# Last two attention levels in smaller places taken by ScalarE, and level halves paired in one half slot

## The chip, the cores and the metric

The kernel runs on one core of one Trainium2 chip. The metric is the device time in microseconds (us) of one execution, the median of several runs. TensorE (PE) multiplies matrices, VectorE (DVE), ScalarE (ACT) and GpSimd (POOL) work elementwise, SyncE (SP) issues the transfers. Each engine takes its instructions in the order in which they are written and waits for semaphores that the other engines raise.

## The reference, cut to what matters

```python
# attention: batch 4, heads 8, seq 768, head_dim 48
f = 1.0 / (1.0 + np.exp(-f_logit))
for t in range(S):
    state = f[:, :, t, :, None] * state + np.einsum('bhd,bhe->bhde', k[:, :, t], v[:, :, t])
    y[:, :, t] = np.einsum('bhd,bhde->bhe', q[:, :, t], state)
# x = y as 3072 tokens x 384; first network, d_ff 2048
h = x @ w_in
g = np.where(h >= 1, h, np.where(h <= -1, 0.0, (h + 1) ** 2 / 4))
x = g @ w_out
# second network, d_ff 1536
g = x @ w_gate
out = (g * sigmoid(g) * (x @ w_val)) @ w2_out
```

All tensors are fp32. The two networks are done with three fp32r products for each fp32 product (hi times hi, hi times lo, lo times hi).

## The kernel before, in words

**Attention.** The sequence is cut into 6 units of 128 steps. The gated recurrence inside a unit is unrolled into a 128x128 matrix of scores for each head, filled in seven levels (`LEVELS`, m = 1, 2, 4 to 64). At level m the queries in the right half of every block of 2m steps meet the keys in its left half. Then the queries of the right half are multiplied by the running gate product (`scale_q`, L731, VectorE), the keys of the left half likewise (`scale_k`, L892, GpSimd), and the gate products of the two halves are merged (`merge`, L900, GpSimd). The 16 pairs of heads go in two groups of 8, so a level has two steps and a unit has 14 (`STEPS`), numbered 0 to 13.

**One step, before.** ScalarE copies the queries of the right halves into `right_q`, one copy for each head of a pair, with zeros between (`copy_right`, L546, two copies of 64x512). TensorE multiplies them with the keys into one PSUM bank of three (`level`, L344, for level 64 L348). VectorE moves the bank into `scores` (`take_level`): for levels 1 to 32 by two masked copies (COPY_PREDICATED, L748), for level 64 by eight small copies (L755). After the levels come four outputs (`outputs`, L370 to L381), and for all units but the last the transposed keys (`turn_keys`, L389), the new state (`key_values`, L400). TensorE may refill a bank when the engine that takes it has done so (`free`).

**The networks.** Unit m of the first network has 16 chunks. A chunk is `hidden` (9 matmuls of 128x512, L431 to L433) and, two chunks later (`LAG`), `project1` (9 matmuls, L445 to L447). Between them VectorE clamps (`clamp`, L818), ScalarE squares (L604), VectorE takes the maximum (`activate`, L825), ScalarE rounds the result to fp32r (`split_g1`, g_hi, L611), and GpSimd subtracts that from it (g_lo, L932). `project1` waits for g_hi and g_lo of its chunk; `hidden(c)` waits until `activate(c-2)` is done.

**The order.** It is written by hand. A chunk c has two half slots: h = 2c lies between `hidden(c)` and the `project1` beside it, h = 2c + 1 behind it. A `Plan` gives the half slots in which each piece of a unit's attention is issued. Unit 0 (`FIRST`) runs alone ahead of the networks, unit 1 (`SECOND`) in unit 0 of the first network, units 2 to 5 (`USUAL`) in its units 1 to 4. Preparations (`own`, `diag`, `place`, `sigmoid`, `gated`) stand in negative half slots, inside the unit before. On VectorE a chunk is: attention of h = 2c, `activate(c-1)`, `clamp(c)`, attention of 2c + 1. On GpSimd: attention of 2c, `split_g1(c-1)`, attention of 2c + 1. The unit of the second network that follows has no attention.

Of the kernel before, what the change touches and what calls it, by code (L numbers as in the profile page):

```python
# [27 lines left out]
STEPS = 2 * NL  # L28
# [9 lines left out]
Y0 = STEPS  # L38
# [12 lines left out]
Plan = namedtuple("Plan", "own diag place sigmoid gated step last_merge y y_out tk tk_out kv state state_place")  # L51
USUAL = Plan(own=(-9, -8), diag=(-8, -7), place=(-6, -5, -4, -3), sigmoid=(-2, -1), gated=(-1, 0),
             step=(1, 3, 5, 7, 8, 9, 10, 12, 13, 14, 15, 17, 18, 19), last_merge=21,
             y=(21, 21, 22, 22), y_out=(21, 22, 22, 23), tk=(23, 23, 24, 24), tk_out=(24, 24, 25, 25),
             kv=25, state=26, state_place=27)
SECOND = Plan(own=(-9, -8), diag=(-8, -7), place=(0, 2, 3, 4), sigmoid=(3, 4), gated=(4, 5),
              step=(6, 8, 9, 10, 11, 12, 13, 14, 16, 17, 18, 19, 20, 21), last_merge=22,
              y=(23, 23, 24, 24), y_out=(23, 24, 24, 25), tk=(25, 25, 26, 26), tk_out=(26, 26, 27, 27),
              kv=27, state=28, state_place=29)
FIRST = USUAL._replace(diag=(-3, -2), sigmoid=(-3, -2), gated=(-3, -2))  # L60
# [7 lines left out]
def steps_at(a, h):  # L68
    return [s for s in range(STEPS) if PLANS[a].step[s] == h]
# [19 lines left out]
def merges(a, s):  # L89

    return sum(STEPS if 0 < b < UNITS - 1 else STEPS - 2 for b in range(a)) + s


def build(nc, f, q, k, qt, kt, v, w_in, w_out, w_gate, w_val, w2_out, masks, ident, x1, out):
# [51 lines left out]
    mask = att("mask", [P, (NL - 1) * HALF // 2], I32)  # L146
# [72 lines left out]
    def _(sp):  # L219
# [71 lines left out]
        sp.wait_ge(dve_took, (UNITS - 1) * DVE_A_UNIT + STEPS)  # L291
# [20 lines left out]
    def _(pe):  # L312
        def free(a, i):

            j = i - 3
            if j < 0:
                a, j = a - 1, FILLS + j
            if a < 0:
                return
            if j < STEPS:  # L320
                pe.wait_ge(dve_took, a * DVE_A_UNIT + j + 1)
            elif j < TK0:
                pe.wait_ge(x_lo_done, a * B + j - Y0 + 1)
# [8 lines left out]
        def level(a, s):  # L332
            li, g = s // 2, s % 2
            free(a, s)
            pe.wait_ge(q_copied, a * STEPS + s + 1)
            if li:
                pe.wait_ge(k_scaled, a * STEPS + s - 1)
            else:
                pe.wait_ge(k_in[g], 16 * (a + 1))
            for x in range(BP // 2):  # L340
                bp = g * BP // 2 + x
                if li < NL - 1:
                    for half in range(2):
                        last = pe.matmul(of(a, s)[rows(half), x * R:(x + 1) * R],  # L344
                                         keys[:, bp, half * HALF:(half + 1) * HALF],
                                         right_q[:, bp, half].rearrange("p e t -> p (e t)"), start=True, stop=True)
                else:
                    last = pe.matmul(of(a, s)[rows(x % 2), x // 2 * P:(x // 2 + 1) * P], keys[:, bp, 0:HALF],  # L348
                                     right_q[:, bp].rearrange("p s e t -> p (s e t)"), start=True, stop=True)
            last.then_inc(filled, 1)  # L350

        def outputs(a, b):
            i = Y0 + b
            free(a, i)
            pe.wait_ge(dve_took, a * DVE_A_UNIT + STEPS - 1 + b // 2)
            if b == 0:
                pe.wait_ge(v_in, 16 * (a + 1))
# [24 lines left out]
            last.then_inc(filled, 1)  # L382

        def turn_keys(a, b):
            i = TK0 + b
            free(a, i)
            pe.wait_ge(k_scaled, a * STEPS + STEPS - 1 + b // 2)
# [16 lines left out]
        def attention(a, h):  # L404
            for s in steps_at(a, h):
                level(a, s)
            for b in range(B):
                if PLANS[a].y[b] == h:
                    outputs(a, b)
# [101 lines left out]
    def _(act):  # L511
# [16 lines left out]
        def copy_right(a, s):  # L528
            li, g = s // 2, s % 2
            act.wait_ge(q_scaled, a * SCALED_A_UNIT + s + 1)  # L530
            if li:
                act.wait_ge(filled, fill(a, s - 1))
            elif a > 0:
                act.wait_ge(filled, fill(a - 1, STEPS))
            for e in range(2):
                o = group(right_q, g)[rows(e), :, :, e, :]
                i = group(queries, g)[rows(e)]
                if li < NL - 1:
                    m = LEVELS[li]
                    i = i.rearrange("p x (h b s r) -> p (x h) b s r", h=2, s=2, r=m)[:, :, :, 1, :]  # L540
                    o = o.rearrange("p x h (b r) -> p (x h) b r", r=m)
                    if m == 1:
                        i, o = i[:, :, :, 0], o[:, :, :, 0]
                else:
                    i = i[:, :, HALF:P].rearrange("p x (s t) -> p x s t", s=2)
# [23 lines left out]
        def attention(a, h):  # L569
# [6 lines left out]
            for s in steps_at(a, h + 1):  # L576
                copy_right(a, s)
            for b in range(B):
                if PLANS[a].y_out[b] == h:
                    split_y(a, b)  # L580
            if a < UNITS - 1:
                for b in range(B):
                    if PLANS[a].tk_out[b] == h:
                        take_keys(a, b)
# [114 lines left out]
    def _(dve):  # L699
# [33 lines left out]
        def take_level(a, s):  # L733
# [9 lines left out]
            if li < NL - 1:  # L743
                m = LEVELS[li]
                for half in range(2):
                    o = group(scores, g)[rows(half), :, :, half * HALF:(half + 1) * HALF]
                    o = o.rearrange("p x e (b s r) -> p (x e) b s r", s=2, r=m)[:, :, :, 1, :]
                    last = dve.copy_predicated(o, level_mask(li, half),  # L748
                                               t[rows(half), :].rearrange("p (x b r) -> p x b r", x=BP, r=m))
            else:  # L750
                for e in range(2):
                    o = group(scores, g)[rows(0), e::2, :, HALF:P].rearrange("p x e (s t) -> p x s e t", s=2)
                    i = t[rows(e), :].rearrange("p (x s e t) -> p x s e t", s=2, e=2, t=HALF // 2)
                    for x in range(BP // 4):
                        last = dve.tensor_copy(o[:, x], i[:, x])  # L755
            last.then_inc(dve_took, 1)

        def decay_state(a):
            dve.wait_ge(g_merged, merges(a, STEPS))
# [22 lines left out]
        def attention(a, h):  # L782
# [7 lines left out]
            for s in steps_at(a, h - 1):  # L790
                take_level(a, s)
            for s in steps_at(a, h):
                scale_q(a, s)
            if h == PLANS[a].last_merge and 0 < a < UNITS - 1:
# [4 lines left out]
            for b in range(B):  # L799
                if PLANS[a].y_out[b] == h:  # L800
                    split_y(a, b)
# [72 lines left out]
    def _(pool):  # L874
# [6 lines left out]
        def scale_k(a, s):  # L881
            li, g = s // 2, s % 2
            m = LEVELS[li]
            pool.wait_ge(filled, fill(a, s + 1))
            if li:
                pool.wait_ge(g_merged, merges(a, s - 1))
                pool.wait_ge(k_scaled, a * STEPS + s - 1)
# [14 lines left out]
        def attention(a, h):  # L902
# [64 lines left out]
def _constants():  # L967
# [4 lines left out]
    for m in LEVELS[:-1]:  # L972
# [62 lines left out]
```

## Time and profile before

| | |
|---|---|
| median of 3 runs | 1078.5 us (1078.38 to 1078.94) |
| the profiled execution's own time | 1078.47 us |
| its span | 1076.7 us |
| PE, share of the span | 94% |
| DVE, ACT, POOL | 51%, 41%, 42% |
| TensorE clock granted, mean | 0.979 |

The span is from the first to the last recorded instruction. Unit 0 of attention lies at about 16 to 78 us. The units 1 to 5 lie beside the first network until about 558 us, then the first network's last unit and the second network follow without attention. A matmul in fp32 is recorded as two passes, so one level step of 16 matmuls shows as x32. A matmul's recorded length includes a tail in which the next one already runs, so what a matmul costs is read from the distance between starts.

### The profile page before, as it was taken

Reading aid. Unit: us, or ns where it says so; the run is one execution under the profiler, and the core shown is the slowest. Engines: PE = TensorE matmul, PEld = TensorE weight load, DVE = VectorE, ACT = ScalarE, POOL = GpSimd, SP = SyncE. Lnnn points to the kernel's source line nnn. Section 1 sums busy time; section 2 is a strip of 40 time slices with the busy share of each in tenths; the row PEclk is TensorE's granted clock in tenths of the full one; section 3 lists DMA queues with packets and bytes.
Section 4 is the critical chain, followed back from the end, with each engine's and each line's share of the span. In section 5 each row is a group of like instructions: output and inputs, shape, how many; then the busy total and the mean of one; then the engine's idle time right before and its main releaser. Section 6 shows DMA issues by size and latency. Waiting matters only on the chain.

```text
span 1076.7 us, 19206 instructions
## 1 busy us (share of the span) xinstructions
PE 1015.5 (94%) x7816; PEld 828.8 (77%) x7816; DVE 547.0 (51%) x745; ACT 445.2 (41%) x808; POOL 450.8 (42%) x368
## 2 busy tenths in 40 slices
PE   2477899999999999999999999999999999999997
PEld 2465677778778777877788888888888888888886
DVE  7965965884686488568736532223222222222221
ACT  3439538544753855375336532122222222222221
POOL 3956962763564476447327422121221212212121
PEclk9569999999999999999999999999999999999999
DMA  9423005003300600220043110010010010000000
GB/s 357 158 72 145 1 2 216 31 2 124 122 1 2 216 30 2 82 107 2 2 177 131 45 39 22 1 59 1 1 59 1 1 59 1 30 1 1 30 1 29
DMA packets 17367, 63.52 MB, mean 59 GB/s; under 512 B 1920, under 2 KB 2176, under 8 KB 16512
## 3 DMA queue, kind: packets, MB, share of 16 engines
q1 hardware_dynamic: 17280, 62.30, 15.8%
q8 instruction: 62, 1.02, 0.4%
q14 instruction: 25, 0.20, 0.1%
HBM read 52.85 MB, written 9.44 MB: 58 GB/s over the span
## 4 chain that ended last, share of the span: by engine, by line
PE 83%; issue 5%; DVE 5%; ACT 3%; POOL 3%; DMA 1%; SPq 0%; POOLq 0%; ACTq 0%; DVEq 0%
PE acc L445 10%; PE acc L447 10%; PE acc L446 10%; PE bank L473 7%; PE bank L471 7%; PE bank L472 7%; PE hid L431 6%; PE bank L344 5%; PE hid L432 5%; PE hid L433 5%; DVE scores L748 3%; PE hid L473 2%; PE hid L472 2%; PE hid L471 2%; PE bank L376 2%
## 5 line engine op out<-in xcount | busy, mean ns | idle before, releaser
L939 POOL TENSOR_TENSOR g_lo<-prod,g_hi 128x512 fp32r<-128x512 f32 x72 | 93.1, 1293 | 347.4 <-ACT g_hi L650 347.4
L932 POOL TENSOR_TENSOR g_lo<-act_tmp,g_hi 128x512 fp32r<-128x512 f32 x96 | 140.5, 1463 | 188.8 <-ACT g_hi L611 188.8
L837 DVE TENSOR_TENSOR sig<-sig,bank 128x512 f32<-128x512 f32 x72 | 49.6, 688 | 275.9 <-ACT sig L644 275.9
L748 DVE COPY_PREDICATED scores<-mask,bank 64x512 f32<-64x512 int32 x144 | 134.2, 932 | 28.4 <-PE bank L344 26.6
L650 ACT CAST g_hi<-prod 128x512 fp32r<-128x512 f32 x72 | 44.9, 624 | 247.6 <-PE acc L447 247.6
L892 POOL TENSOR_TENSOR keys<-keys,gates 128x512 f32<-128x512 f32 x82 | 110.2, 1343 | 44.1 <-PE bank L344 32.7
L611 ACT CAST g_hi<-act_tmp 128x512 fp32r<-128x512 f32 x96 | 59.6, 621 | 164.1 <-DVE act_tmp L825 164.1
L344 PEld LDWEIGHTS bank<-right_q,keys 128*64 128x64 f32 x2304 | 81.0, 150 | 58.8 <-issue 54.6
L344 PE MATMUL bank<-right_q,keys 128*64 128x64 f32 x2304 | 91.0, 238 | 36.0 <-ACT right_q L546 28.1
L445 PE MATMUL acc<-g_hi,wout_hi 128*128 128x512 f32 x288 | 117.0, 406 | 8.0 <-POOL g_lo L932 8.0
L431 PE MATMUL hid<-x_hi,win_hi 128*128 128x512 f32 x288 | 119.0, 413 | 4.0 <-DVE act_tmp L825 4.0
L546 ACT COPY right_q<-queries 64x512 f32<-64x512 f32 x168 | 105.8, 630 | 40.7 <-DVE queries L731 22.5
L433 PE MATMUL hid<-x_hi,win_lo 128*128 128x512 f32 x288 | 113.1, 393 | 0.0
L432 PE MATMUL hid<-x_lo,win_hi 128*128 128x512 f32 x288 | 113.0, 393 | 0.0
L446 PE MATMUL acc<-g_lo,wout_hi 128*128 128x512 f32 x288 | 112.7, 391 | 0.0
L447 PE MATMUL acc<-g_hi,wout_lo 128*128 128x512 f32 x288 | 112.5, 391 | 0.0
L731 DVE TENSOR_TENSOR queries<-queries,gates 128x512 f32<-128x512 f32 x84 | 88.3, 1051 | 2.2 <-ACT right_q L546 0.5
L825 DVE TENSOR_TENSOR act_tmp<-hid,act_tmp 128x512 f32<-128x512 f32 x96 | 66.1, 689 | 41.3 <-ACT act_tmp L604 39.8
L445 PE MATMUL acc<-g_hi,wo_hi 128*128 128x512 f32 x216 | 84.1, 389 | 0.2 <-POOL g_lo L939 0.2
L446 PE MATMUL acc<-g_lo,wo_hi 128*128 128x512 f32 x216 | 84.0, 389 | 0.0
L471 PE MATMUL bank<-x_hi,wg_hi 128*128 128x512 f32 x216 | 84.0, 389 | 0.0
L472 PE MATMUL bank<-x_lo,wg_hi 128*128 128x512 f32 x216 | 84.0, 389 | 0.0
(80 smaller groups left out, 1851.6 us busy)
## 6 DMA issues: line engine op xcount, KB each, us to landing
gates<-in_f_dram SPq DMA_DIRECT2D x12, 512.0 KB, 5.3
queries<-in_q_dram SPq DMA_DIRECT2D x12, 512.0 KB, 5.4
keys<-in_k_dram SPq DMA_DIRECT2D x12, 512.0 KB, 4.7
values<-in_v_tok_dram SPq DMA_DIRECT2D x6, 1024.0 KB, 8.8
q_tok<-in_q_tok_dram SPq DMA_DIRECT2D x12, 384.0 KB, 8.6
k_tok<-in_k_tok_dram SPq DMA_DIRECT2D x12, 384.0 KB, 9.0
x_dram<-x_out SPq DMA_DIRECT2D x6, 768.0 KB, 3.9
x_raw<-x_dram SPq DMA_DIRECT2D x6, 768.0 KB, 5.5
```

The lines of the kernel that those rows point to most:

```text
L344: last = pe.matmul(of(a, s)[rows(half), x * R:(x + 1) * R], keys[:, bp, half * HALF:(half + 1) * HALF], right_q[:, bp, half].rearrange("p ...
L431: pe.matmul(o, hi, x_hi[m % 2][:, kc], start=(kc == 0), stop=False)
L432: pe.matmul(o, hi, x_lo[m % 2][:, kc], start=False, stop=False)
L433: last = pe.matmul(o, lo, x_hi[m % 2][:, kc], start=False, stop=(kc == KC - 1))
L445: pe.matmul(o, hi, g_hi[:, c % RING], start=first, stop=False)
L446: pe.matmul(o, hi, g_lo[:, c % RING], start=False, stop=False)
L447: last = pe.matmul(o, lo, g_hi[:, c % RING], start=False, stop=last_chunk)
L471: pe.matmul(o[c % 2][:, :], hi, x_hi[u % 2][:, kc], start=(kc == 0), stop=False)
L472: pe.matmul(o[c % 2][:, :], hi, x_lo[u % 2][:, kc], start=False, stop=False)
L748: last = dve.copy_predicated(o, level_mask(li, half), t[rows(half), :].rearrange("p (x b r) -> p x b r", x=BP, r=m))
L892: pool.tensor_tensor(kl, kl, right.broadcast_to([P, BP // 2 * P // (2 * m), m]), ALU.mult).then_inc(k_scaled, 1)
L932: pool.tensor_tensor(g_lo[:, c % RING, :], act_tmp[:, 2 + c % 2, :], g_hi[:, c % RING, :].bitcast(F32), ALU.subtract).then_inc(g_lo_done, 1)
```

## The change

Three things change together.

1. **Level 32 in one place** (`whole`). Both groups of heads go into one bank, with only the 32 left keys of each half as weights (32 columns), four column quarters side by side. No mask is needed, and ScalarE takes the bank by four copies of 32 rows (`take_whole`).
2. **Level 64 without `right_q`** (`last_level`). Each head is its own matmul with 64 rows of keys and the queries read directly, into two banks. ScalarE takes them by two copies each (`take_last`). The two copies of the queries for each step are gone, and `scale_q` and `scale_k` of these two steps wait for the matmuls.
3. **The order.** A plan names copies, takes, scalings and GpSimd work apart. For units 2 to 5 steps 0 and 1 stand in one half slot (2), 2 and 3 in 5, 4 and 5 in 8, 6 and 7 in 11, 8 and 9 in 13; level 32 is in 16 and level 64 in 18. The outputs begin at 21 as before. `merge` no longer waits for `scale_q`.

TensorE's 14 blocks of levels for a unit from the third on become 7, unit 1's become 12, with the networks' matmuls between.

```diff
-USUAL = Plan(own=(-9, -8), diag=(-8, -7), place=(-6, -5, -4, -3), sigmoid=(-2, -1), gated=(-1, 0),
-             step=(1, 3, 5, 7, 8, 9, 10, 12, 13, 14, 15, 17, 18, 19), last_merge=21,
+ALONE = usual((1, 3, 5, 7, 8, 9, 10, 12, 13, 14), 16, 18, 21)
+USUAL = usual((2, 2, 5, 5, 8, 8, 11, 11, 13, 13), 16, 18, 21,
+              copy=(0, 1, 3, 4, 6, 7, 9, 10, 12, 12, 15, 15), take=(3, 4, 6, 7, 9, 10, 12, 13, 14, 15))
+SECOND = usual((6, 8, 9, 10, 11, 12, 13, 14, 16, 17), 19, 21, 23, place=(0, 2, 3, 4), sigmoid=(3, 4), gated=(4, 5))
...
+        def whole(a):
+
+            free(a, WHOLE0)
+            pe.wait_ge(q_copied, (a + 1) * COPIES)
+            pe.wait_ge(k_scaled, a * SCALES + STEPS)
+            for x in range(BP):
+                for half in range(2):
+                    q = 2 * half + x % 2
+                    last = pe.matmul(of(a, WHOLE0)[Q * q:Q * (q + 1), x // 2 * R:(x // 2 + 1) * R],
+                                     keys[:, x, half * HALF:half * HALF + Q],
+                                     right_q[:, x, half].rearrange("p e t -> p (e t)"), start=True, stop=True)
+            last.then_inc(filled, 1)
+
+        def last_level(a):
+
+            for e in range(2):
+                free(a, LAST0 + e)
+            pe.wait_ge(q_scaled, a * SCALED_A_UNIT + SCALES)
+            pe.wait_ge(k_scaled, a * SCALES + SCALES - 2)
+            for x in range(BP):
+                for e in range(2):
+                    last = pe.matmul(of(a, LAST0 + e)[rows(x % 2), x // 2 * HALF:(x // 2 + 1) * HALF],
+                                     keys[rows(e), x, 0:HALF], queries[rows(e), x, HALF:P], start=True, stop=True)
+            last.then_inc(filled, 2)
...
+        def take_whole(a):
+            act.wait_ge(filled, fill(a, LAST0))
+            act.wait_ge(dve_took, a * DVE_A_UNIT + STEPS)
...
+                    last = act.copy(o, i)
+            last.then_inc(act_took, 1)
+
+        def take_last(a, e):
+            act.wait_ge(filled, fill(a, Y0))
+            act.wait_ge(dve_took, a * DVE_A_UNIT + STEPS)
...
         def scale_q(a, s):
...
-            dve.wait_ge(q_copied, a * STEPS + s + 1)
+            if s < COPIES:
+                dve.wait_ge(q_copied, a * COPIES + s + 1)
+            else:
+                dve.wait_ge(filled, fill(a, Y0))
...
         def scale_k(a, s):
...
-            pool.wait_ge(filled, fill(a, s + 1))
+            if s < STEPS:
+                pool.wait_ge(filled, fill(a, s + 1))
+            else:
+                pool.wait_ge(filled, fill(a, LAST0 if s < COPIES else Y0))
...
         def merge(a, s):
...
-            pool.wait_ge(k_scaled, a * STEPS + s + 1)
-            pool.wait_ge(q_scaled, a * SCALED_A_UNIT + 2 + s + 1)
+            pool.wait_ge(k_scaled, a * SCALES + s + 1)
```

On GpSimd, at the first level of unit 2 (L892 and L954 are `scale_k`, L900 and L961 `merge`, L932 and L993 the g_lo of a chunk). Before:

```order
L892 TENSOR_TENSOR keys<-keys,gates 128x512
L900 TENSOR_TENSOR gates<-gates 128x512
L932 TENSOR_TENSOR g_lo<-act_tmp,g_hi 128x512
L892 TENSOR_TENSOR keys<-keys,gates 128x512
L900 TENSOR_TENSOR gates<-gates 128x512
L932 TENSOR_TENSOR g_lo<-act_tmp,g_hi 128x512
```

And now:

```order
L954 TENSOR_TENSOR keys<-keys,gates 128x512
L961 TENSOR_TENSOR gates<-gates 128x512
L954 TENSOR_TENSOR keys<-keys,gates 128x512
L961 TENSOR_TENSOR gates<-gates 128x512
L993 TENSOR_TENSOR g_lo<-act_tmp,g_hi 128x512 x2
```

Both scalings and both merges stand ahead of the g_lo of the chunk.

On VectorE, at the last levels of unit 2 (L731 and L798 are `scale_q`, L748 the masked and L755 the plain take, L825 and L884 `activate`, L818 and L877 `clamp`). Before:

```order
L825 TENSOR_TENSOR act_tmp<-hid,act_tmp 128x512
L818 TENSOR_SCALAR act_tmp<-hid 128x512
L731 TENSOR_TENSOR queries<-queries,gates 128x16x32
L748 COPY_PREDICATED scores<-mask,bank 64x16x32 x2
L731 TENSOR_TENSOR queries<-queries,gates 128x8x64
L825 TENSOR_TENSOR act_tmp<-hid,act_tmp 128x512
L818 TENSOR_SCALAR act_tmp<-hid 128x512
L755 COPY scores<-bank 64x2x2x32 x8
L731 TENSOR_TENSOR queries<-queries,gates 128x8x64
L755 COPY scores<-bank 64x2x2x32 x8
L825 TENSOR_TENSOR act_tmp<-hid,act_tmp 128x512
```

And now:

```order
L798 TENSOR_TENSOR queries<-queries,gates 128x16x32 x2
L884 TENSOR_TENSOR act_tmp<-hid,act_tmp 128x512
L877 TENSOR_SCALAR act_tmp<-hid 128x512
L798 TENSOR_TENSOR queries<-queries,gates 128x8x64 x2
L884 TENSOR_TENSOR act_tmp<-hid,act_tmp 128x512
L877 TENSOR_SCALAR act_tmp<-hid 128x512
```

The takes are gone from here, and both scalings of level 64, which now wait for its matmuls, stand ahead of an `activate`.

## Rows read from the trace of the kernel before

**Rows 1.** Busy time of stretches; columns: stretch, length, busy us by engine.

```profile
17.00:76.00 59.00, 33.63 (x568) 30.52 (x564) 51.82 (x62) 26.75 (x42) 45.93 (x36) 0.65 0.38 147
278.60:374.60 96.00, 95.01 (x1009) 75.93 (x1008) 67.93 (x98) 53.94 (x108) 52.91 (x47) 1.00 0.20 70
648.00:1076.00 428.00, 423.19 (x1866) 349.77 (x1864) 102.60 (x142) 99.10 (x160) 89.22 (x69) 1.00 0.05 17
```

**Rows 2.** What PE waited for in 182.5 to 278.6 us: total, times, longest.

```profile
PE acc L445 <- POOL g_lo L932: 1.0, 2, 0.6
```

**Rows 3.** PE in order of time, levels of unit 3: start, us, line, tile.

```profile
301.93 1.15 PE L344 MATMUL bank<-right_q,keys 128*64 128x64 f32 x32
303.01 0.50 PE L445 MATMUL acc<-g_hi,wout_hi 128*128 128x512 f32 x1
...
305.28 1.15 PE L344 MATMUL bank<-right_q,keys 128*64 128x64 f32 x32
...
308.62 1.15 PE L344 MATMUL bank<-right_q,keys 128*64 128x64 f32 x32
...
314.01 1.15 PE L344 MATMUL bank<-right_q,keys 128*64 128x64 f32 x32
```

**Rows 4.** PE in order of time, level 64, outputs, state of unit 3.

```profile
336.07 1.09 PE L348 MATMUL bank<-right_q,keys 128*64 128x128 f32 x16
...
342.95 0.84 PE L370 MATMUL bank<-queries,state_apart 128*32 128x128 f32 x24
343.61 0.84 PE L376 MATMUL bank<-scores,values 128*32 128x128 f32 x24
...
358.23 2.07 PE L400 MATMUL bank<-values,keys_tok 128*64 128x48 f32 x64
```

**Rows 5.** Chain of waits, 350 to 360 us: start, us on the chain.

```profile
352.42 0.87 PE bank L389 x8
```

**Rows 6.** POOL in order of time, unit 3.

```profile
284.04 1.53 POOL L892 TENSOR_TENSOR keys<-keys,gates 128x512 f32<-128x512 f32 x1
285.65 1.04 POOL L900 TENSOR_TENSOR gates<-gates 128x512 f32<-128x512 f32 x1
...
303.18 1.28 POOL L892 TENSOR_TENSOR keys<-keys,gates 128x512 f32<-128x512 f32 x1 [0.77 <-PE bank L344]
304.54 0.66 POOL L900 TENSOR_TENSOR gates<-gates 128x128 f32<-128x128 f32 x1
305.15 1.28 POOL L932 TENSOR_TENSOR g_lo<-act_tmp,g_hi 128x512 fp32r<-128x512 f32 x1
...
333.97 1.06 POOL L892 TENSOR_TENSOR keys<-keys,gates 128x512 f32<-128x512 f32 x1 [1.88 <-PE bank L348]
335.11 0.22 POOL L900 TENSOR_TENSOR gates<-gates 128x8 f32<-128x8 f32 x1
335.29 1.75 POOL L932 TENSOR_TENSOR g_lo<-act_tmp,g_hi 128x512 fp32r<-128x512 f32 x1
```

**Rows 7.** DVE in order of time, unit 3.

```profile
283.62 2.68 DVE L748 COPY_PREDICATED scores<-mask,bank 64x512 f32<-64x512 int32 x2 [0.70 <-PE bank L344]
...
332.18 0.69 DVE L731 TENSOR_TENSOR queries<-queries,gates 128x512 f32<-128x512 f32 x1
332.90 0.69 DVE L825 TENSOR_TENSOR act_tmp<-hid,act_tmp 128x512 f32<-128x512 f32 x1
...
335.81 1.77 DVE L731 TENSOR_TENSOR queries<-queries,gates 128x512 f32<-128x512 f32 x1
```

**Rows 8.** ACT groups by line: count, busy, mean ns.

```profile
L611 ACT CAST g_hi<-act_tmp 128x512 fp32r<-128x512 f32 x96 | 59.6, 621 | 164.1 <-DVE act_tmp L825 164.1
...
L556 ACT COPY keys_tok<-bank 128x512 f32<-128x512 f32 x20 | 10.7, 588 | 3.2 <-PE bank L389 3.1
```

**Rows 9.** PE in order of time, end of unit 0.

```profile
53.85 1.97 PE L344 MATMUL bank<-right_q,keys 128*64 128x64 f32 x32 [0.98 <-issue]
56.61 1.97 PE L348 MATMUL bank<-right_q,keys 128*64 128x128 f32 x16 [0.79 <-ACT right_q L546]
63.40 1.98 PE L348 MATMUL bank<-right_q,keys 128*64 128x128 f32 x16 [4.82 <-POOL keys L892]
67.37 1.51 PE L376 MATMUL bank<-scores,values 128*32 128x128 f32 x24 [2.00 <-DVE queries L731]
```

**Rows 10.** DVE, ACT and POOL in order of time, end of unit 0.

```profile
55.26 1.48 DVE L748 COPY_PREDICATED scores<-mask,bank 64x512 f32<-64x512 int32 x2
...
63.84 1.81 DVE L755 COPY scores<-bank 64x128 f32<-64x128 f32 x8
...
52.50 1.25 ACT L546 COPY right_q<-queries 64x512 f32<-64x512 f32 x2 [0.84 <-DVE queries L731]
...
56.44 3.57 POOL L879 TENSOR_TENSOR q_tok<-q_tok,k_tok 128x768 f32<-128x768 f32 x2
```

More of the change, by code:

```diff
@@ L33 @@
 PIECE = 2 * DM
-Y0 = STEPS
+WHOLE0 = STEPS
+LAST0 = WHOLE0 + 1
+Y0 = LAST0 + 2
 TK0 = Y0 + B
@@ L65, with placed @@
 Q = P // 4
-def steps_at(a, h):
-    return [s for s in range(STEPS) if PLANS[a].step[s] == h]
+def placed(places, h):
+    return [i for i, p in enumerate(places) if p == h]
 def turns(m, h):
@@ L89, in merges @@
 def merges(a, s):
-    return sum(STEPS if 0 < b < UNITS - 1 else STEPS - 2 for b in range(a)) + s
+    return sum(SCALES if 0 < b < UNITS - 1 else SCALES - 2 for b in range(a)) + s
 def build(nc, f, q, k, qt, kt, v, w_in, w_out, w_gate, w_val, w2_out, masks, ident, x1, out):
@@ L341, in level @@
                 bp = g * BP // 2 + x
[L342 to L349, printed above, removed]
-            last.then_inc(filled, 1)
+                for half in range(2):
+                    last = pe.matmul(of(a, s)[rows(half), x * R:(x + 1) * R],
+                                     keys[:, bp, half * HALF:(half + 1) * HALF],
+                                     right_q[:, bp, half].rearrange("p e t -> p (e t)"), start=True, stop=True)
+            last.then_inc(filled, 1)
+        def whole(a):
[3 more added lines that the diff above has]
+            for x in range(BP):
+                for half in range(2):
+                    q = 2 * half + x % 2
[13 more added lines that the diff above has]
+            last.then_inc(filled, 2)
         def outputs(a, b):
@@ L404, in attention @@
         def attention(a, h):
-            for s in steps_at(a, h):
+            for s in placed(PLANS[a].step, h):
                 level(a, s)
-            for b in range(B):
-                if PLANS[a].y[b] == h:
-                    outputs(a, b)
+            if h == PLANS[a].whole:
+                whole(a)
+            if h == PLANS[a].last:
+                last_level(a)
+            for b in placed(PLANS[a].y, h):
+                outputs(a, b)
             if a < UNITS - 1:
@@ L533, in copy_right @@
             elif a > 0:
-                act.wait_ge(filled, fill(a - 1, STEPS))
+                act.wait_ge(filled, fill(a - 1, LAST0))
             for e in range(2):
[L536 to L545, printed above, removed]
+                o = group(right_q, g)[rows(e), :, :, e, :].rearrange("p x h (b r) -> p (x h) b r", r=m)
+                i = group(queries, g)[rows(e)].rearrange("p x (h b s r) -> p (x h) b s r", h=2, s=2, r=m)[:, :, :, 1, :]
+                if m == 1:
+                    i, o = i[:, :, :, 0], o[:, :, :, 0]
                 last = act.copy(o, i)
             last.then_inc(q_copied, 1)
+        def take_whole(a):
+            act.wait_ge(filled, fill(a, LAST0))
+            act.wait_ge(dve_took, a * DVE_A_UNIT + STEPS)
+            t = bank[fill(a, WHOLE0) % 3]
+            for half in range(2):
+                for par in range(2):
+                    q = 2 * half + par
+                    o = scores[half * HALF:half * HALF + Q, par::2, :, half * HALF + Q:(half + 1) * HALF]
+                    i = t[Q * q:Q * (q + 1), :].rearrange("p (x e t) -> p x e t", e=2, t=Q)
+                    last = act.copy(o, i)
[3 more added lines that the diff above has]
+            act.wait_ge(dve_took, a * DVE_A_UNIT + STEPS)
+            t = bank[fill(a, LAST0 + e) % 3]
+            for par in range(2):
+                last = act.copy(scores[rows(0), par::2, e, HALF:P], t[rows(par), :].rearrange("p (x t) -> p x t", t=HALF))
+            last.then_inc(act_took, 1)
         def take_keys(a, b):
@@ L575, in attention @@
                     sigmoid(a, g)
-            for s in steps_at(a, h + 1):
+            if h == PLANS[a].whole_take:
+                take_whole(a)
+            if h == PLANS[a].last_take:
+                for e in range(2):
+                    take_last(a, e)
+            for s in placed(PLANS[a].copy, h):
                 copy_right(a, s)
-            for b in range(B):
-                if PLANS[a].y_out[b] == h:
-                    split_y(a, b)
+            for b in placed(PLANS[a].y_out, h):
+                split_y(a, b)
             if a < UNITS - 1:
-                for b in range(B):
-                    if PLANS[a].tk_out[b] == h:
-                        take_keys(a, b)
+                for b in placed(PLANS[a].tk_out, h):
+                    take_keys(a, b)
                 if h == PLANS[a].state_place:
@@ L742, in take_level @@
                 dve.wait_ge(mask_in, 16)
[L743 to L755, printed above, removed]
+            m = LEVELS[li]
+            for half in range(2):
+                o = group(scores, g)[rows(half), :, :, half * HALF:(half + 1) * HALF]
+                o = o.rearrange("p x e (b s r) -> p (x e) b s r", s=2, r=m)[:, :, :, 1, :]
+                last = dve.copy_predicated(o, level_mask(li, half),
+                                           t[rows(half), :].rearrange("p (x b r) -> p x b r", x=BP, r=m))
             last.then_inc(dve_took, 1)
         def decay_state(a):
-            dve.wait_ge(g_merged, merges(a, STEPS))
+            dve.wait_ge(g_merged, merges(a, SCALES))
             dve.wait_ge(state_placed, 2 * a)
@@ L789, in attention @@
                     gated(a, g)
-            for s in steps_at(a, h - 1):
+            for s in placed(PLANS[a].take, h):
                 take_level(a, s)
-            for s in steps_at(a, h):
+            for s in placed(PLANS[a].scale, h):
                 scale_q(a, s)
-            if h == PLANS[a].last_merge and 0 < a < UNITS - 1:
+            if h == PLANS[a].decay and 0 < a < UNITS - 1:
                 decay_state(a)
@@ L798, in attention @@
                     add_state(a, g)
-            for b in range(B):
-                if PLANS[a].y_out[b] == h:
-                    split_y(a, b)
+            for b in placed(PLANS[a].y_out, h):
+                split_y(a, b)
         def split_w2(i):
@@ L971, in _constants @@
     parts = []
-    for m in LEVELS[:-1]:
+    for m in LEVELS[:-2]:
         right = i[:, (i[0] // m) % 2 == 1]
```

56 lines of the change are left out of this document (32 added, 24 removed).

## The prediction, made before the result was known

> **What bounds the kernel now.** I read the busy time by stretches first. Where attention and the first network run together, TensorE is busy 95.01 of 96.00 us; in the second network 423.19 of 428.00; only unit 0 of attention, at 17 to 76 us, has it busy 33.63 of 59.00, at a granted clock of 0.65, with VectorE at 51.82 [rows 1]. So there are two kernels in one: a start bound by VectorE and the chain through it, and a long stretch in which every microsecond that TensorE's order needs is a microsecond of the end. Then I read what TensorE waits for in a usual unit: 1.0 us in two waits for g_lo of GpSimd [rows 2]. Engines other than TensorE cost there only if they make it wait, and each of them has room on average. TensorE's own sequence came next [rows 3 to 5], last the engines that release it [rows 6 to 8].
>
> **Switching blocks on TensorE.** Two levels with 9 large matmuls between start 305.28 - 301.93 = 3.35 us apart, with 18 between 314.01 - 308.62 = 5.39, so 9 large matmuls cost 2.04 and a level in its place 1.31. From its start to the next large matmul it is 303.01 - 301.93 = 1.08 [rows 3]. The other 0.23 us is paid for going from one kind of matmul to the other and back, once for a block. Two levels side by side should pay it once. That is this change's gain: 7 blocks fewer in each of units 2 to 5, 7 x 4 x 0.23 = 6.4 us, and 2 fewer in unit 1, 0.5 us. Together -6.9 us.
>
> The trace shows a price for the switch. The Trainium skill's page "TensorEngine Tiling (Array Packing)", Key Properties, says that a change of tiling mode drains the engine while another tile of the same mode does not; by that rule too the price goes with the block, and the trace agrees (0.23 us).
>
> **The matmuls themselves.** A level step is 32 passes in 1.08 us, 34 ns each [rows 3]. Level 32 was 2 x 1.08 = 2.16 us and is now 64 passes of 32 columns. The nearest rows with 32 columns are 24 passes in 343.61 - 342.95 = 0.66 us, 27 ns [rows 4], so 1.7 to 2.2 us; I take no change. Level 64 was 2 steps of x16; the row of one is 1.09 with its tail [rows 4], so about 2.1 us for both. It is now 64 passes of 64 rows by 64 columns. Narrow passes of x64 took 2.07 us [rows 4], 31 to 34 ns each whatever they hold, so 2.0 to 2.2: no change. What the trace doesn't show is whether two matmuls on different row halves and the same columns overlap. If not, each costs half of a full pass of 128 columns (0.87 / 8 = 109 ns [rows 5]), 54 ns, so 64 x 54 = 3.5 us, +1.4 a unit; that is the upper end. If four quarters ran wholly side by side, 64 x 13.6 = 0.9 us, -1.2 a unit, the lower end. I take the middle since that is where rows of narrow passes lie.
>
> **Unit 0, alone.** VectorE loses four takes, about 2 x 1.48 + 2 x 1.81 = 6.6 us [rows 10]. I don't count them as gain, for other things become late. `whole` needs the copies of steps 10 and 11; the second comes after `scale_q` of step 9, as in the row that ends at 52.50 + 1.25 = 53.75 [rows 10]. At that stretch's clock a pass costs 1.97 / 32 = 62 ns [rows 9], so 64 passes end at 53.75 + 3.9 = 57.7. Then GpSimd scales keys for both groups (2 x (1.06 + 0.22) = 2.6, to 60.3), for the last level waits for it [rows 6]; the level takes 3.9 (64.2), and ScalarE's four copies 4 x 0.59 = 2.4 [rows 8], so the outputs may start at 66.6, against 67.37 [rows 9]: -0.8 us. In the same place GpSimd's two products of 3.57 us for unit 1 [rows 10] are now split around step 10, and VectorE's sum of the second stands before `scale_q` of step 12; that ends by about 66.4 as well, so it's no later. Bounds: at full clock both blocks are 2.2 instead of 3.9 us, -4 us; if row halves don't overlap at this clock, +2.9 more.
>
> **What the change makes late in units 2 to 5.** Three places. I set each against the time at which TensorE would arrive.
>
> *Half slot 2.* GpSimd does `scale_k`, `merge`, `scale_k`, `merge` ahead of g_lo of chunk 0. From the end F of step 0: 2 x (1.53 + 1.04 + 0.08 between) = 5.3, then g_lo 1.28 [rows 6], with 0.1 for the handing over: F + 6.7. TensorE after F: step 1 and project with its switch 3.35 - 0.08, then `hidden(2)` 2.04: F + 5.3. It waits 1.4 us. Before, one `scale_k` and one `merge` stood there. The scalings took 1.53 beside masked copies (2.68 us [rows 7]) and 1.06 to 1.28 elsewhere [rows 6]; by 1.28 the wait is 0.9. Upper end 1.7, by a g_lo of 1.6. Queued behind the late project are the pair of slot 5 and the rest of TensorE, so it is paid in full.
>
> *Half slot 8.* The same with 1.28 and 0.66: 2 x (1.28 + 0.66 + 0.08) + 1.28 + 0.1 = 5.4, against 5.3. Some scalings are longer here, so I take 0.3; ends 0 and 0.8. Slots 5, 11 and 13 are odd, there g_lo of the chunk stands ahead of the pair, and slot 16 has the level of slot 18 behind it before its project: nothing.
>
> *Half slot 18.* `scale_q` of steps 12 and 13 used to wait for copies only. Now they wait for the end L of level 64, and `activate(8)` is behind them, for which `hidden(10)` waits. TensorE gets there at L + 2.2 (one project and its switch). VectorE: 0.69 + 0.69 + 0.69 = 2.1 if undisturbed [rows 7]. But GpSimd starts `scale_k` at the same L. The trace shows what that does: `scale_q` took 1.77 us beside a g_lo of 1.75, and 0.69 alone [rows 6, 7]. With one of GpSimd's 1.06 between the two, `activate` ends at L + 3.1, so `hidden(10)` waits 0.9. Then ScalarE's rounding 0.62 [rows 8] and g_lo 1.28 give L + 5.5 where project comes at L + 5.2: 0.3 more. Together 1.2, ends 0 and 1.7. In unit 5 GpSimd has nothing to do for the last level, so only some 0.15 is left.
>
> The Trainium skill's "GPSIMD Engine Reference", Specifications, says that GpSimd shares its SBUF interfaces with VectorE and contends with VectorE instructions that have two SBUF inputs; `scale_q` has two. The rows agree (1.77 against 0.69 us). Without such contention slot 18 would cost near nothing and the sum would be some 3 us lower, so this rule speaks against the change.
>
> Sum of waits: 3 x (1.4 + 0.3 + 1.2) + (1.4 + 0.3 + 0.15) = 10.5 us. Removed: on GpSimd the wait of `merge` for `scale_q`, at nothing, for both engines were held by the same contention there. ScalarE gets 8 copies for 4; it has 42 us of room in 96 [rows 1], and its takes end before slot 21. The transfer of the masks is shorter, hidden.
>
> **Sum.** -6.9 - 0.8 + 10.5 = +2.8. The profiled execution took 1078.47 us, 0.03 under the median, so 1081.3.
>
> **Rivals.**
> *B, faster.* GpSimd is quicker now that the masked copies lie in other half slots: 1.28 for scalings, slot 8 free, slot 18 at 0.3. Then waits are 4 x 0.9 + 3 x 0.3 = 4.5, and the sum is -6.9 - 0.8 + 4.5 = -3.2: 1075.3. For it: scalings of 1.06 occur [rows 6]. Against: at levels 1 and 2 the masked copies still follow at once. It decides when the pair with its g_lo takes under 6.2 us instead of 6.7.
> *C, a wash.* The wait behind slot 2 is half of what I give it, since the scaling of one group may run before the masked copy beside it starts: -4 x 0.7, so 1078.5.
> *D, slower still.* The row halves of level 64 don't overlap: 5 x 1.4 + 2.9 = +9.9 on the forecast, 1091. For it: same columns one behind the other. Against: nothing shown.
> *E, the last level at a quarter.* 5 x -1.2 - 2 = -8: 1073. Against it the 31 ns floor of narrow passes [rows 4]. The Trainium skill's tiling page, Theoretical Speedup, allows four times where both dimensions are at most 64; this would be its effect.
> *F, no saving.* The 0.23 belongs to each bank filled, not to the block: 1081.3 + 6.9 = 1088. Against: x64 in one block took 2.07 [rows 4], no more for each pass than x32.
>
> **Chances.** Forecast 0.40, B 0.24, C 0.20, D 0.07, E 0.04, F 0.05. The range runs from 1073 to 1087. The forecast's own is 1079.5 to 1084. About 2.2 us (0.2%) is what a measurement can tell; the cases give faster 0.29, same 0.24, slower 0.47.
>
> **What will show it.** Right: pairs of levels as x64 in about 2.2 us; TensorE waiting for g_lo 1 to 1.6 us behind slot 2 of units 2 to 5 and for act_tmp behind level 64; unit 0's outputs starting at 66 to 67 us; a usual unit of about 97.4 us for 96.0. Wrong: a usual unit under 96; level 64's block far from 2.1 us; unit 0 shorter by over 3 us.

## The result and the profile after

The changed kernel took 1069.07 us (median of 6 runs, 1068.19 to 1070.0), the kernel before in the same comparison 1078.44 us. The ratio is 0.9912 with a 95% interval of 0.9899 to 0.9925: 0.9% faster. The prediction was 1081.3 us, slower, with a range from 1073 to 1087. The time lies outside it, on the other side.

The profiled execution took 1068.27 us (span 1066.5). First the busy time of the two stretches that answer to [rows 1], one usual unit being 94.92 us long where it was 96.0:

```profile
17.00:76.00 59.00, 31.12 (x642) 28.60 (x639) 46.97 (x44) 29.18 (x46) 46.73 (x36) 0.83 0.42 158
283.99:378.91 94.92, 91.65 (x1041) 74.04 (x1040) 59.47 (x78) 56.42 (x112) 51.41 (x47) 1.00 0.20 71
```

TensorE's busy time in a unit fell from 95.01 to 91.65 us, by 3.4, while the unit became only 1.1 shorter. So TensorE has less to do and waits more. What it waited for in one unit, 278 to 373 us (who, for whom, total, times, longest), against 1.0 us in [rows 2]:

```profile
PE acc L491 <- POOL g_lo L993: 2.7, 4, 1.5
PE hid L477 <- DVE act_tmp L884: 0.6, 1, 0.6
```

TensorE in order of time in that unit, against [rows 3, 4]. L364 is a level of two halves, L377 level 32 (`whole`), L390 level 64 (`last_level`), L491 a project and L477 a hidden; in brackets the idle time before and who ended it:

```profile
278.46 2.08 PE L364 MATMUL bank<-right_q,keys 128*64 128x64 f32 x64
280.47 0.50 PE L491 MATMUL acc<-g_hi,wout_hi 128*128 128x512 f32 x1
...
286.33 0.47 PE L491 MATMUL acc<-g_hi,wout_hi 128*128 128x512 f32 x1 [1.48 <-POOL g_lo L993]
...
303.60 0.47 PE L491 MATMUL acc<-g_hi,wout_hi 128*128 128x512 f32 x1 [0.25 <-POOL g_lo L993]
...
320.52 1.10 PE L377 MATMUL bank<-right_q,keys 128*32 128x64 f32 x64
321.55 0.50 PE L491 MATMUL acc<-g_hi,wout_hi 128*128 128x512 f32 x1
...
325.85 1.16 PE L390 MATMUL bank<-queries,keys 64*64 64x64 f32 x64
326.94 0.50 PE L491 MATMUL acc<-g_hi,wout_hi 128*128 128x512 f32 x1
...
329.89 0.50 PE L477 MATMUL hid<-x_hi,win_hi 128*128 128x512 f32 x1 [0.61 <-DVE act_tmp L884]
```

The three waits that the prediction placed are there: 1.48, 0.25 and 0.61 us, where it gave 1.4, 0.3 and 0.9. What it did not have is in the starts: level 32 takes 321.55 - 320.52 = 1.03 us for 64 passes, level 64 takes 326.94 - 325.85 = 1.09. That is 16 and 17 ns a pass, where the prediction took 31 to 34.

The wait behind slot 2 on GpSimd, both scalings (L954) and merges (L961) ahead of g_lo (L993), as the order said:

```profile
279.70 1.53 POOL L954 TENSOR_TENSOR keys<-keys,gates 128x512 f32<-128x512 f32 x1 [1.62 <-PE bank L364]
281.31 1.04 POOL L961 TENSOR_TENSOR gates<-gates 128x512 f32<-128x512 f32 x1
282.31 1.53 POOL L954 TENSOR_TENSOR keys<-keys,gates 128x512 f32<-128x512 f32 x1
283.91 1.04 POOL L961 TENSOR_TENSOR gates<-gates 128x512 f32<-128x512 f32 x1
284.91 1.27 POOL L993 TENSOR_TENSOR g_lo<-act_tmp,g_hi 128x512 fp32r<-128x512 f32 x1
```

The end of unit 0 on TensorE, against [rows 9]. The outputs (L419) start 2.1 us earlier (65.23 for 67.37), and the two small levels take some 1.9 us each at this place, not 3.9. The granted clock of 50 to 63 us is 0.50 (1.2 GHz) in both profiles:

```profile
53.62 1.94 PE L377 MATMUL bank<-right_q,keys 128*32 128x64 f32 x64 [5.60 <-ACT right_q L587]
59.36 1.99 PE L390 MATMUL bank<-queries,keys 64*64 64x64 f32 x64 [3.80 <-POOL keys L954]
65.23 1.51 PE L419 MATMUL bank<-scores,values 128*32 128x128 f32 x24 [3.89 <-DVE queries L798]
```

Not all of the 2.1 us is the change. The first block of levels, TensorE's first matmuls, starts at 16.36 us in the kernel before and at 15.81 in the changed one:

```profile
16.36 1.97 PE L344 MATMUL bank<-right_q,keys 128*64 128x64 f32 x32 [16.36 <-ACT right_q L546]
15.81 1.97 PE L364 MATMUL bank<-right_q,keys 128*64 128x64 f32 x32 [15.81 <-ACT right_q L587]
```

In the experiments below whose unit 0 is the changed kernel's (4 to 8) this start lies between 16.18 and 16.44 us. From it to the outputs it is 51.01 us before, 49.42 in the changed kernel and 49.40 to 49.47 in those five, so 1.6 us is what the change gives there, and 0.55 us is an earlier start that it doesn't explain.

By the starts of each unit's state (L400, L443), the 10.2 us between the two profiled executions are: unit 0 2.1 (75.60 to 73.51), unit 1 2.7 (94.87 to 92.19 us long), units 2 to 4 1.2 each, and what is left, 1.9, in unit 5 and behind it.

### The profile page after: what moved, and what is told of

Same layout as the page of the kernel before. It is cut to its first block, busy times and chain, and to the rows that moved or that the text cites. A ratio compares the mean times of both kernels' runs of the same rounds, so it can differ in the third digit from the quotient of the medians.

```text
span 1066.5 us, 19376 instructions
## 1 busy us (share of the span) xinstructions
PE 994.6 (93%) x8008; PEld 816.0 (77%) x8008; DVE 502.3 (47%) x625; ACT 458.4 (43%) x832; POOL 446.1 (42%) x368
## 4 chain that ended last, share of the span: by engine, by line
PE 78%; POOL 10%; issue 6%; ACT 3%; DVE 2%; DMA 1%; SPq 0%; POOLq 0%; ACTq 0%; DVEq 0%
PE acc L491 10%; PE acc L493 9%; PE acc L492 9%; PE bank L517 7%; PE bank L518 7%; PE bank L519 7%; PE hid L477 5%; PE hid L479 4%; PE hid L478 4%; POOL keys L954 4%; PE bank L364 4%; POOL g_lo L993 3%; PE hid L517 2%; PE hid L519 2%; PE hid L518 2%
## 5 line engine op out<-in xcount | busy, mean ns | idle before, releaser
L993 POOL TENSOR_TENSOR g_lo<-act_tmp,g_hi 128x512 fp32r<-128x512 f32 x96 | 134.0, 1397 | 166.8 <-ACT g_hi L675 166.8
L954 POOL TENSOR_TENSOR keys<-keys,gates 128x512 f32<-128x512 f32 x82 | 109.5, 1336 | 65.2 <-PE bank L364 43.8
L491 PE MATMUL acc<-g_hi,wout_hi 128*128 128x512 f32 x288 | 117.2, 407 | 14.8 <-POOL g_lo L993 14.8
L814 DVE COPY_PREDICATED scores<-mask,bank 64x512 f32<-64x512 int32 x120 | 116.1, 967 | 15.9 <-PE bank L364 14.4
L477 PE MATMUL hid<-x_hi,win_hi 128*128 128x512 f32 x288 | 116.9, 406 | 5.7 <-DVE act_tmp L884 5.7
L587 ACT COPY right_q<-queries 64x512 f32<-64x512 f32 x144 | 90.8, 631 | 43.9 <-PE bank L364 21.8
L364 PE MATMUL bank<-right_q,keys 128*64 128x64 f32 x1920 | 71.0, 236 | 32.2 <-ACT right_q L587 26.0
L364 PEld LDWEIGHTS bank<-right_q,keys 128*64 128x64 f32 x1920 | 65.5, 149 | 44.2 <-issue 41.4
L798 DVE TENSOR_TENSOR queries<-queries,gates 128x512 f32<-128x512 f32 x84 | 81.3, 995 | 29.9 <-PE bank L390 25.5
L884 DVE TENSOR_TENSOR act_tmp<-hid,act_tmp 128x512 f32<-128x512 f32 x96 | 65.9, 687 | 52.7 <-ACT act_tmp L668 51.6
L877 DVE TENSOR_SCALAR act_tmp<-hid 128x512 f32<-128x512 f32 x96 | 65.7, 685 | 47.0 <-PE hid L479 47.0
L491 PE MATMUL acc<-g_hi,wo_hi 128*128 128x512 f32 x216 | 84.1, 389 | 0.2 <-POOL g_lo L1000 0.2
L493 PE MATMUL acc<-g_hi,wo_lo 128*128 128x512 f32 x216 | 84.0, 389 | 0.0
```

What stands on the lines that cost most here:

```text
L364: last = pe.matmul(of(a, s)[rows(half), x * R:(x + 1) * R], keys[:, bp, half * HALF:(half + 1) * HALF], right_q[:, bp, half].rearrange("p ...
L477: pe.matmul(o, hi, x_hi[m % 2][:, kc], start=(kc == 0), stop=False)
L491: pe.matmul(o, hi, g_hi[:, c % RING], start=first, stop=False)
L493: last = pe.matmul(o, lo, g_hi[:, c % RING], start=False, stop=last_chunk)
L814: last = dve.copy_predicated(o, level_mask(li, half), t[rows(half), :].rearrange("p (x b r) -> p x b r", x=BP, r=m))
L954: pool.tensor_tensor(kl, kl, right.broadcast_to([P, BP // 2 * P // (2 * m), m]), ALU.mult).then_inc(k_scaled, 1)
```

## The experiments

Each kernel is the changed one with the edit shown. Its time stands beside the changed kernel's 1069.07; ratios are to the kernel before in the same comparison.

**1. Level 32 on one quarter after the other.**

```diff
-            for x in range(BP):
-                for half in range(2):
+            for half in range(2):
+                for x in (*range(0, BP, 2), *range(1, BP, 2)):
```

> Level 32 in all six units with its 32 matmuls in another order: eight in a row on the same quarter of the columns. Same instructions, same sizes. Theory A (a pass holds its quarter for about 64 ns, and the block takes 16 ns a pass only because four quarters run side by side): the block takes about 64 x 64 ns = 4.1 us for 1.03, +3.1 in five units and more in unit 0: about 1085. Theory B (a pass with 32 columns of weights is cheap in itself, by its short weight load): no change, 1069.

Measured 1080.72 us, ratio 1.002 (1.001 to 1.003): the whole gain is gone. The block on TensorE:

```profile
327.14 3.18 PE L377 MATMUL bank<-right_q,keys 128*32 128x64 f32 x64
330.25 0.50 PE L491 MATMUL acc<-g_hi,wout_hi 128*128 128x512 f32 x1
```

It takes 3.11 us, 49 ns a pass, for the same instructions in another order. A unit is 96.9 us for 94.9. Theory B falls. Theory A stands, with a pass of 49 ns instead of my 64, so four quarters side by side gave three times, not four.

**2. Level 64 on one half of the rows after the other.**

```diff
-            for x in range(BP):
-                for e in range(2):
+            for e in range(2):
+                for x in range(BP):
                     last = pe.matmul(of(a, LAST0 + e)[rows(x % 2), x // 2 * HALF:(x // 2 + 1) * HALF],
```

> Level 64 in all units with its 32 matmuls in another order: first all on rows 0 to 63, then all on rows 64 to 127, so that only two of the four quarters of the array follow each other. Theory A (side by side is what makes it cheap): the block costs 32 ns a pass as the levels of two halves do, 2.0 us for 1.09, +0.9 in five units and up to 1.8 in unit 0, of which units 2 to 4 hide nothing: about 1074. Theory B (64 rows of weights instead of 128 are cheap in themselves): no change, 1069.

Measured 1073.03 us (0.9955, 0.994 to 0.997). The block takes 330.88 - 329.04 = 1.84 us, 29 ns a pass:

```profile
329.04 1.91 PE L390 MATMUL bank<-queries,keys 64*64 64x64 f32 x64
330.88 0.50 PE L491 MATMUL acc<-g_hi,wout_hi 128*128 128x512 f32 x1
```

As theory A has it: with both row halves in turn the block costs 17 ns a pass, with one 29. One thing goes along with the row half and was not tested apart: the two row halves fill different banks, so in the changed kernel each matmul goes to another bank than the one ahead of it, and in this experiment 16 in a row go to one. In experiment 1 all 32 matmuls fill one bank, and there it is the quarters alone.

**3. Both levels near the price of the prediction.** The edit of experiment 2, and for level 32 `for x in (*range(0, BP, 2), *range(1, BP, 2))` with the halves inside, which alternates between two quarters.

> The changed kernel with both small levels in an order in which only two quarters of the array follow each other: level 32 alternates between column quarters 0 and 2, then 1 and 3; level 64 is all on rows 0 to 63, then on 64 to 127. That is the price the prediction gave these levels (about 2.1 us each for 1.03 and 1.09). Theory A (the price of the two levels is the term that was wrong, the others hold): a unit is 94.9 + 0.75 (seen with level 64 alone) + 0.6 to 1.0 = 96.3 to 96.7, and the time 1076 to 1080. Rival (something else in the changed kernel gave the gain): under 1074.

Measured 1075.89 us (0.9974, 0.9965 to 0.9984), just under the interval I gave; the rival asked for under 1074. Level 32 takes 326.31 - 324.58 = 1.73 us, level 64 again 1.84:

```profile
324.58 1.79 PE L377 MATMUL bank<-right_q,keys 128*32 128x64 f32 x64
326.31 0.50 PE L491 MATMUL acc<-g_hi,wout_hi 128*128 128x512 f32 x1
```

A unit takes 96.35 us, 0.3 more than before the change, so with two quarters at a time the change is close to nothing in units 2 to 4. 6.8 us of the gain of 9.4 hang on the order of the matmuls inside two blocks.

**4. One step in each half slot again.**

```diff
-USUAL = usual((2, 2, 5, 5, 8, 8, 11, 11, 13, 13), 16, 18, 21, ...)
+USUAL = usual((1, 3, 5, 7, 8, 9, 10, 12, 13, 14), 16, 18, 21)
```

> Units 2 to 5 with one step in each half slot again (1, 3, 5, 7, 8, 9, 10, 12, 13, 14), levels 32 and 64 as changed. Theory A (the gain is the two small levels, 16 and 17 ns a pass where 31 to 34 was paid; pairing pays back in waits for g_lo what it saves in switches): five more blocks and single levels cost 13.1 - 11.2 = 1.9 us a unit, the waits of 1.5 and 0.25 us behind slots 2 and 8 go, so 4 x 0.15 = +0.6 on the changed kernel, 1068.9 to 1070. Theory B (pairing is the gain, since the waits would come with any order): +1.9 x 4 = +7.6, near 1076.

Measured 1067.08 us (0.9891, 0.9877 to 0.9904). I had expected 1068.9 to 1070 by theory A, so that is missed too, on the fast side. The 2.0 us to the changed kernel are hardly more than the times alone can tell (the intervals of the two ratios overlap a little); the length of a unit is the better witness, 94.47 us for 94.90. The waits of 1.48 and 0.25 are gone, the one of 0.61 stays. Pairing as the change does it costs more than it saves, some 0.4 us a unit; theory B falls. I had missed that a wait costs some 0.2 us more than its idle time: without the wait the matmul at 286.33 would have started 0.23 after the one at 284.46, so it is 1.64 late, and its successor comes 0.30 behind it instead of 0.23.

**5. Only the first pair into an odd slot.**

```diff
-USUAL = usual((2, 2, 5, 5, 8, 8, ...), ..., take=(3, 4, 6, 7, ...))
+USUAL = usual((3, 3, 5, 5, 8, 8, ...), ..., take=(4, 5, 6, 7, ...))
```

> Only steps 0 and 1 of units 2 to 5 move from half slot 2 to 3 (their takes to 4 and 5). Theory A (the 1.5 us wait for g_lo exists because slot 2 puts two scalings and two merges ahead of g_lo of that chunk on GpSimd, and an odd slot puts them behind): the wait goes, 4 x 1.5 = -6.0, about 1063. Theory B (GpSimd is simply short of time at the start of a unit, the wait only moves to the next chunk or to the pair in slot 5, which now comes 2 half slots later): no change, 1069.

Measured 1072.87 us (0.9945, 0.9931 to 0.9958): slower. The wait for g_lo behind the first pair is gone, as A has it. But the one behind slot 8 grew from 0.25 to 0.71 us (at 306.72), TensorE now waits 1.72 us for VectorE as well, and the unit is 95.8 us long:

```profile
297.32 0.50 PE L477 MATMUL hid<-x_hi,win_hi 128*128 128x512 f32 x1 [1.72 <-DVE act_tmp L884]
```

VectorE's order there says why. Two masked takes (L814) of 2.7 us each and two scalings between them stand in a row, and the `activate` (L884) that hidden waits for is behind them:

```profile
288.79 2.68 DVE L814 COPY_PREDICATED scores<-mask,bank 64x512 f32<-64x512 int32 x2
291.51 2.35 DVE L798 TENSOR_TENSOR queries<-queries,gates 128x512 f32<-128x512 f32 x2
293.89 2.66 DVE L814 COPY_PREDICATED scores<-mask,bank 64x512 f32<-64x512 int32 x2
296.58 0.69 DVE L884 TENSOR_TENSOR act_tmp<-hid,act_tmp 128x512 f32<-128x512 f32 x1
```

So both theories missed: the time is not what either gave, and most of the wait is now one for another engine. The new order made this wait; it wasn't there behind the old one. In the changed kernel the four masked copies stand in one row without scalings, and the `activate` behind them ends at 285.87, 4.7 us ahead of the `hidden` at 290.60 that needs it:

```profile
279.76 5.40 DVE L814 COPY_PREDICATED scores<-mask,bank 64x512 f32<-64x512 int32 x4
285.18 0.69 DVE L884 TENSOR_TENSOR act_tmp<-hid,act_tmp 128x512 f32<-128x512 f32 x1
```

**6. All pairs odd, level 64 in slot 19.**

```diff
+USUAL = usual((3, 3, 5, 5, 9, 9, 11, 11, 13, 13), 16, 19, 21,
+              copy=(0, 1, 3, 4, 6, 7, 10, 10, 12, 12, 15, 15), take=(4, 5, 6, 7, 10, 11, 12, 13, 14, 15))
```

> As before, and also steps 4 and 5 in slot 9 and level 64 in slot 19 of units 2 to 5, so that only level 32 is left in an even slot. Theory A: the waits behind slots 2, 8 and 18 all go, 4 x (1.5 + 0.25) + 3 x 0.6 and 0.3 for g_lo in unit 5 = -9, about 1060. Theory B (they move): 1067 to 1069. A rival in between: level 64 in slot 19 leaves ScalarE 2 half slots for its takes before the outputs at 21, and these become the wait: 1063.

Measured 1068.0 us (0.9899, 0.9886 to 0.9913), a unit of 94.5 us for 94.9. The waits for g_lo behind the pairs and the one behind level 64 are gone; the one for VectorE is the only large one left (1.75 us at 294.85, and so in each of the four units), with 0.3 us before level 32. The result alone would have spoken for theory B; the waits show that it was right only for the first two pairs.

**7. Experiment 4 with level 64 in slot 19.** `USUAL = usual((1, 3, 5, 7, 8, 9, 10, 12, 13, 14), 16, 19, 21)`.

> The unpaired order with level 64 in slot 19 instead of 18 of units 2 to 5. Theory A (the wait of 0.61 us and its restart of some 0.2 come from the scalings of queries that wait for level 64 ahead of an activate; behind an odd slot the activate of that chunk stands ahead of them): 0.84 x 3 less than unpaired's 1067.1, 1064.6. Rival (ScalarE's four takes of 2.4 us then come too late for the outputs in slot 21): no gain or worse, 1067 to 1069.

Measured 1064.77 us (0.9875, 0.9859 to 0.9891). A unit is 93.8 us for 94.5, and TensorE has no wait for VectorE in it. The scalings ahead of `activate` were the cause, and ScalarE's takes are in time.

**8. Singles first, then pairs in odd slots.**

```diff
+USUAL = usual((1, 3, 5, 7, 9, 9, 11, 11, 13, 13), 17, 19, 21,
+              copy=(0, 2, 4, 6, 7, 8, 10, 10, 12, 12, 15, 15), take=(2, 4, 6, 8, 10, 11, 12, 13, 14, 15))
```

> Steps 0 to 3 (levels 1 and 2, whose masked takes cost VectorE 2.7 us each) alone in slots 1, 3, 5, 7, then pairs in 9, 11, 13, level 32 in 17, level 64 in 19: no scaling in an even slot. Theory A (a pair saves 0.38 us where neither g_lo nor activate is held up by it; the 1.5 us of the changed kernel and the 1.7 us of the order with pairs in 3 and 5 are GpSimd's and VectorE's queues, not the pair's price): a unit of 94.47 - 3 x 0.38 - 0.84 = 92.5 us, with four units about 1060. Rival (pairs in 9, 11 and 13 leave copies or takes late, and waits of 1 to 2 us come up there): 1066 to 1069.

Measured 1059.65 us (0.9832, 0.9818 to 0.9847): 9 us under the changed kernel, 18.5 under the kernel before in its own comparison (1078.1). A unit is 92.4 us, and the only waits left in it are the two at its start that the kernel before had too:

```profile
PE acc L491 <- POOL g_lo L993: 0.9, 2, 0.6
```

Its pairs on TensorE follow at 6.32 us, 2 half slots of 2.04 and 2.24 for the pair:

```profile
295.65 2.08 PE L364 MATMUL bank<-right_q,keys 128*64 128x64 f32 x64
301.97 2.08 PE L364 MATMUL bank<-right_q,keys 128*64 128x64 f32 x64
308.29 2.08 PE L364 MATMUL bank<-right_q,keys 128*64 128x64 f32 x64
```

Two single levels cost 2.62 [rows 3], so a pair saves 0.38 where nothing waits.

**9. The wait of merge back in.** `pool.wait_ge(q_scaled, a * SCALED_A_UNIT + 2 + s + 1)` in `merge`.

> The changed kernel with the wait of merge for scale_q put back. Theory A (it costs nothing: in units 2 to 5 scale_q is done long before, and in units 0 and 1 the two engines exclude each other there anyway): 1068 to 1070. Rival (part of unit 0's gain of 2.1 us comes from it, since GpSimd idles 0.7 us at four merges in the profile before): +1 to +2, 1070 to 1071.

Measured 1069.09 us (0.9918, 0.9903 to 0.9933), the changed kernel's own time, and a unit is 94.91 us as there. Unit 0's outputs start 49.42 us after the first block, as in the changed kernel. That part of the change does nothing that these runs can tell.

## Why the prediction was wrong

**The step that failed** is in "The matmuls themselves": "Narrow passes of x64 took 2.07 us [rows 4], 31 to 34 ns each whatever they hold", and so "no change" for both small levels. I read the 31 to 34 ns as a floor for any pass. Those rows are all passes of 64 columns, of which two fit side by side. What the runs show in its place is that the time of a pass depends on how many parts of the array follow each other in turn. For level 32 it is 49 ns with one quarter (experiment 1), 27 with two (experiment 3) and 16 with four; for level 64 it is 29 with two (experiment 2) and 17 with four. Level 32 fell by 2.16 - 1.03 = 1.1 us a unit and level 64 by about 1.0 where I wrote zero. The row of 27 ns for passes of 32 columns, which I took as the nearest, already had its four quarters in turn (`place` in `outputs`), but 128 columns of queries for 64 here; that this is why it took 27 and not 16 is likely, and not tested. The runs show that the order decides. Whether the passes queue at their part of the array or at the rows of the bank that it fills they can't tell, for a column quarter always fills its own rows.

The same error was in rival E, which had the right mechanism: its ground against it was the floor, it was priced for level 64 alone, and it had a chance of 0.04.

The Trainium skill's page "TensorEngine Tiling (Array Packing)", Theoretical Speedup, gives up to twice for a dimension of at most 64 and up to four times for one of at most 32. That was nearer than my reading: for level 32, with 32 columns, experiment 1 shows 49 / 16 = 3 times from four parts. The four times of rival E is the table's twice for each of two dimensions, worked out from it and not one of its lines; level 64 went from 29 ns with two parts to 17 with four, 1.7 times.

**Switches** (0.23 us a block): right. It left out that the second level of a pair costs 0.94 and not 1.08 us (2.02 for the pair), another 0.7 a unit.

**Waits**: placed right, sized nearly right. Slot 2: 1.4 forecast, 1.48 measured; slot 8: 0.3 and 0.25; slot 18: 0.9 for `activate` and 0.61, and the 0.3 for g_lo behind it did not come. In unit 5 the wait of slot 18 is absent; I had left 0.15 for it. With some 0.2 each by which a wait costs more than its idle time (experiment 4) they cost 3.0 us a unit where 2.9 was forecast. That these agree is in part luck: the 0.2 was not in the forecast, and it stands where the 0.3 and the missing part of the 0.9 stood.

**A usual unit together**: switches -1.6, pairs -0.7, levels 32 and 64 -2.1, waits +3.0, in sum -1.4; the trace has -1.15. With zero for the second and the third term the same sum gives +1.4, which is the forecast's unit of 97.4 us for 96.0.

**Unit 0**: -0.8 forecast, -2.1 measured, of which 1.6 is the change and 0.55 the earlier start. The two levels took 1.9 us for the forecast's 3.9 each, but more than half of those 4 us is no gain. In experiment 3 they take 3.02 and 3.08 us there, and the outputs still start 66.46 - 17.03 = 49.43 us after the first block:

```profile
54.83 3.02 PE L377 MATMUL bank<-right_q,keys 128*32 128x64 f32 x64 [5.61 <-ACT right_q L587]
60.59 3.08 PE L390 MATMUL bank<-queries,keys 64*64 64x64 f32 x64 [2.74 <-POOL keys L954]
66.46 1.51 PE L419 MATMUL bank<-scores,values 128*32 128x128 f32 x24 [2.80 <-DVE queries L798]
```

So the last 1.1 us of each is hidden: behind level 32 by GpSimd, whose key scaling stands behind the product for unit 1, and behind level 64 by VectorE's sum of the second product. The forecast had the outputs wait for ScalarE's takes; they waited for `scale_q`. **Unit 1**: -0.5 forecast, -2.7 measured; the two levels again account for 2.1 of it, if they save there what they save in a usual unit.

**The total**: experiment 3 puts back most of the price that I had assumed and has 1075.9 us. So of the 12.2 us between 1081.3 and 1069.1, 6.8 are shown to be this term. The other 5.4 were not tested apart. By the traces the cheaper pairs are worth 4 x 0.7 = 2.8, what even that order saves against my 2.16 and 2.1 (1.73 and 1.84 us) about 5 x 0.7 = 3.5, and unit 0 0.8. That comes to 7.1, so the account closes to some 2 us and no better.

## What to carry to other kernels

Before a measured time per small matmul is used as a floor, see how many parts of the array followed in turn in that row, and count how many the new code has in turn; the order of the loop decides it. A pair of steps is only cheaper if the work that it puts in a row on the other engines doesn't stand ahead of something that TensorE needs within the next block: look at which side of that instruction the pair lands, and pair the cheap steps, not the costly ones. When an order is changed to take one wait away, look at once at what the new order puts in a row on the other engines: experiment 5 took away 1.48 us for GpSimd and made 1.72 for VectorE.

## What the runs showed of the hardware that was not expected

The same 64 passes of level 32 take 1.03, 1.73 or 3.11 us with four, two or one quarter in turn. In unit 0 kernels with the same instructions there differ by up to 1.1 us: the state starts at 73.39 us in experiment 4 and at 74.45 in experiment 5. The granted clock of the profile doesn't explain it. At 17 to 76 us it was 0.83 for the changed kernel, 0.65 in experiment 5 and 1.00 (2.4 GHz all along) in experiment 9:

```profile
17.00:76.00 59.00, 31.18 (x639) 28.72 (x638) 47.02 (x43) 29.18 (x46) 46.70 (x36) 0.65 0.40 153
17.00:76.00 59.00, 33.01 (x653) 30.39 (x650) 47.30 (x43) 29.21 (x46) 46.13 (x36) 1.00 0.41 157
47.27 1.97 PE L364 MATMUL bank<-right_q,keys 128*64 128x64 f32 x32 [1.86 <-ACT right_q L587]
```

But under that 1.00 a level of 32 passes still took 1.97 us (the last line, experiment 9), as long as in the kernel before under 0.50 (53.85 in [rows 9]) and not the 1.15 of the later units; and the state of experiment 9 starts at 73.96, later than the changed kernel's 73.51. So in unit 0 the recorded clock does not tell how long the passes take; why stays open. Part of the differences lies ahead of TensorE's first matmul, at 15.81 us in the changed kernel, 16.44 in experiment 5 and 16.52 in experiment 9. For comparisons of 1 to 2 us the length of a usual unit, where the granted clock is 1.00 and a level takes 1.15 us, is the better measure.
